# A fused attention and two-MLP kernel: q and k transposed by VectorE instead of TensorE, and w_out's two halves kept in DRAM

## Chip, cores and metric

The kernel runs on one core of a Trainium2 chip. The metric is device time in microseconds (us), the median of several executions; lower is better.

## The reference

```python
# attention: B=4, H=8, S=768, D=64; n_global=8, n_local=96
scores = scale * q @ k.T                       # per batch and head
rel = pos[:, None] - pos[None, :]
keep = (pos[None, :] < n_global) | ((rel >= 0) & (rel < n_local))
scores = where(keep, scores - slope[h] * dist, -1e9)
a = softmax(scores)                            # over keys
x = (a @ v)  -> reshaped to [B*S = 3072 tokens, H*D = 512]
# first MLP, 512 -> 2048 -> 512
h = x @ moe_w_in;  y = (h * cos(h)) @ moe_w_out
# second MLP, 512 -> 2048 -> 512
h = maximum(y @ moe2_w_in, 0);  out = (h * h) @ moe2_w_out
```

All arrays are float32. A query sees at most 96 keys behind it and the first 8 keys of the sequence.

## The kernel before

**Attention** is done in 48 groups. `place(G)` gives each group's batch `b`, its run `r` of 256 positions (three in a sequence) and its pair `j` of heads; four groups (the four pairs of heads) share a run. For a group, `load_qk` brings 256 rows of q and k for two heads with four DMAs into `raw`, positions on the partitions. TensorE turns them with four transposes of 128x128 into PSUM (`transpose_qk`, L593), and ScalarE copies the result into `kq` (`copy_qk`, L759), which holds for each pair of heads the first 8 keys, the 96 keys that precede the run, the run's 256 keys and its 256 queries, head dimension on the partitions. Before a run is overwritten, GpSimd moves the last 96 keys to the front (`move_tail`, L480); `copy_qk` waits for that (`tails_moved`). When `r` is 0 there is nothing to move, and ScalarE copies the first 8 keys to their places (L761).

Then, group by group: `scores` (TensorE, L615), `reduces` (VectorE, L962: adds the bias, takes the row's extreme), `exps` (ScalarE, L771), `invert` (VectorE, L968 and L970: one over the row sums), `normalise` (GpSimd, L487), `turn_probs` (TensorE, L633 and L636), `copy_probs` (ScalarE and VectorE, L741 to L743), `attend` (TensorE, L651), `round_x` (ScalarE, L786) and `low_x` (VectorE, L981). The last two split the result into a high and a low part for the MLP.

**The MLPs** work on six tiles of 512 tokens each. Both matrices and both activations are split in two (high, low), and each product is made from three matmuls. A step F is one block of 128 hidden units of one tile: `up(F)` has 12 matmuls (L557 to L559) and `down(F)` 12 (L576 to L578 in the first MLP, L581 to L583 in the second). There are 96 steps in each MLP, 16 in a tile. Between up and down, ScalarE copies the hidden block (`front`), VectorE computes angles (`angle`, L997 to L1003, first MLP only), ScalarE takes the sine, VectorE gates (`gate`), ScalarE rounds (`round_g`, L812) and VectorE forms the low part (`low_g`, L1017). GpSimd splits each step's 128 rows of w_out (`split_out`, L472 and L474) into one of three slots, anew for each tile, after a DMA of 256 KB (`load_w_out`); it waits until the down step that read the slot is done. In the first steps it also splits w_in (`split_in`, L463 and L465), and later the second MLP's w_in (`split_w2`), which goes through DRAM.

**Order.** Every engine's queue is written out by hand and runs in order; engines meet at semaphores. A prologue does the first 11 groups (`AHEAD`), a loop over G on each engine. GpSimd's loop is: `move_tail(G + 1)`, `normalise(G - 1)`, `split_in(G)` for G below 5 (`EARLY`). VectorE's is: `reduces(G)`, `biases(G + 1)` for the first few, `invert(G - 1)`, `copy_probs(G - 2)`, `low_x(G - 3)`. ScalarE's is: `copy_qk(G + 1)`, `exps(G)`, `copy_probs(G - 2)`, `round_x(G - 3)`. Then come pairs p of steps, F = 2p, in which the work of the groups G = p + 11 is woven, until p = 48. All DMAs are issued by SP, in order; a DMA whose wait isn't met holds up those behind it.

The program takes this path when n_local and n_global fit (here they do); a general path stands beside it.

Of the kernel before, what the change touches and what calls it, by code (L numbers as in the profile page):

```python
# [22 lines left out]
def build(nc, q, k, v, n_global, n_local, w1_in, w1_out, w2_in, w2_out, out):  # L23
# [39 lines left out]
    w2_dram = nc.dram_tensor("w2_dram", (FC, P, 2, KC, P), F32, kind="Internal").ap()  # L63
    y_dram = nc.dram_tensor("y_dram", (KC, P, TOK), F32, kind="Internal").ap()

    with ExitStack() as ctx:
# [17 lines left out]
        raw = sb("raw", [P, 3, 2, 2, 2 * D])  # L84
# [15 lines left out]
        with ExitStack() as lay:  # L100
            x_parts = [sb(f"x_parts{i}", [P, 2, KC, NT], F32R, lay) for i in range(2)]
            w_stage = sb("w_stage", [P, 2, KC, P], F32, lay)
            w_out_raw = sb("w_out_raw", [P, 2, DM], F32, lay)
            w_out_hi = sb("w_out_hi", [P, 3, DM], F32R, lay)
            w_out_lo = sb("w_out_lo", [P, 3, DM], F32R, lay)
# [36 lines left out]
        def turn_bank(G):  # L142
            return 6 if G <= AHEAD else 5

# [32 lines left out]
        qk_transposed = sem("qk_transposed")  # L177
        tails_moved = sem("tails_moved")
        qkT_copied = sem("qkT_copied")
# [21 lines left out]
        w_out_hi_ready = sem("w_out_hi_ready")  # L201
        w_out_ready = sem("w_out_ready")
# [29 lines left out]

        def tails(G):
            return sum(place(n)[1] > 0 for n in range(G + 1))

# [27 lines left out]
        def _(sp):  # L263
# [55 lines left out]
            def load_w_out(F):  # L319
                src, f = (w1_out if F < STEPS else w2_out), F % FC  # L320
                if F >= 2:
                    sp.wait_ge(w_out_ready, F - 1)
                sp.dma_start(w_out_raw[:, F % 2], src[P * f:P * f + P, :]).then_inc(w_out_loaded[F % 2], 16)

# [25 lines left out]
            def pair(p, window):  # L350
                F, G = 2 * p, p + AHEAD
                i, s = divmod(p, FC // 2)
                if window and G + 3 < GROUPS:
                    load_qk(G + 3)
                if window and G + 1 < GROUPS:
                    load_values(G + 1)
                for n in (F + 1, F + 2):
                    if STEPS - FC <= n < STEPS:
                        place_w2(n - (STEPS - FC))
                if W2_FROM <= p < W2_FROM + 2 * FC:  # L360
                    n, late = divmod(p - W2_FROM, 2)
# [12 lines left out]
                if F + 5 < STEPS_ALL:  # L374
                    load_w_out(F + 5)

# [26 lines left out]
            def general():  # L403
                sp.wait_ge(qk_loaded[0], 64)
# [33 lines left out]
        def _(pool):  # L438
# [28 lines left out]
            def split_out(F):  # L467
                pool.wait_ge(w_out_loaded[F % 2], 16 * (F // 2 + 1))
                if F >= 3:
                    pool.wait_ge(down_done, KC * (F - 2))  # L470
                row, hi, lo = w_out_raw[:, F % 2], w_out_hi[:, F % 3], w_out_lo[:, F % 3]
                pool.tensor_scalar(hi, row, 1.0, 1.0, ALU.mult, ALU.mult).then_inc(w_out_hi_ready, 1)  # L472
                pool.wait_ge(w_out_hi_ready, F + 1)
                pool.tensor_tensor(lo, row, hi.bitcast(F32), ALU.subtract).then_inc(w_out_ready, 1)  # L474
# [28 lines left out]
            def window():  # L503
                for G in range(AHEAD):
# [3 lines left out]
                    if G < EARLY:  # L508
                        split_in(G)
                normalise(AHEAD - 1)  # L510
# [9 lines left out]
            def general():  # L520
                pool.wait_ge(mask_steps, MASK_STEPS)
                pool.wait_ge(qk_loaded[0], 64)
# [16 lines left out]
        def _(pe):  # L539
# [22 lines left out]
            def down(F, window):  # L562
                i, f = divmod(F, FC)
                pe.wait_ge(w_out_ready, F + 1)
# [5 lines left out]
                for c in range(KC):  # L570
# [3 lines left out]
                    if i < TILES:  # L574
                        hi, lo = w_out_hi[:, F % 3, cols], w_out_lo[:, F % 3, cols]
# [3 lines left out]
                    else:  # L579
                        hi, lo = g_hi[:, F % 3, cols], g_lo[:, F % 3, cols]  # L580
                        pe.matmul(to, hi, w_out_hi[:, F % 3], start=one, stop=False)  # L581
                        pe.matmul(to, hi, w_out_lo[:, F % 3], start=False, stop=False)  # L582
                        last = pe.matmul(to, lo, w_out_hi[:, F % 3], start=False, stop=end)  # L583
                    last.then_inc(down_done, 1)

            def transpose_qk(G):
                pe.wait_ge(qk_loaded[G % 3], 64 * (G // 3 + 1))
                if 0 < G <= AHEAD:
                    pe.wait_ge(qkT_copied, G)
                if G > AHEAD:  # L590
                    pe.wait_ge(x_lo_ready, G - 2)
                for n in range(4):
                    last = pe.transpose(psum[:, turn_bank(G), P * n:P * n + P], raw[:, G % 3, n // 2, n % 2], ident[:])  # L593
                last.then_inc(qk_transposed, 1)

            def scores(G):
                b, r, j = place(G)
                pe.wait_ge(qkT_copied, G + 1)
# [40 lines left out]
            def attend(G):  # L639
# [4 lines left out]
                if 0 < G < AHEAD - 1:  # L644
                    pe.wait_ge(x_lo_ready, G)
# [11 lines left out]
            def pair(p, window):  # L657
# [8 lines left out]
                if window and G + 1 < GROUPS:  # L666
                    transpose_qk(G + 1)
# [8 lines left out]
            def window():  # L676
                transpose_qk(0)
                for G in range(AHEAD - 1):
                    scores(G)
                    transpose_qk(G + 1)  # L680
# [6 lines left out]
                transpose_qk(AHEAD)  # L687
# [61 lines left out]
        def _(act):  # L749

            def copy_qk(G):
                b, r, j = place(G)
                act.wait_ge(qk_transposed, G + 1)
                if r > 0:
                    act.wait_ge(tails_moved, tails(G))
                elif G >= PAIRS:
                    act.wait_ge(scores_ready, 2 * (G - PAIRS + 1))
                ends = kq[:, j, BACK:Q_AT + 2 * P].rearrange("p (a n) -> p a n", a=2)[:, :, GLOB:]
                last = act.copy(ends, psum[:, turn_bank(G)].rearrange("p (a n) -> p a n", a=2))  # L759
                if r == 0:  # L760
                    last = act.copy(kq[:, j].rearrange("p (a n) -> p a n", a=2)[:, :, 0:GLOB],  # L761
                                    psum[:, turn_bank(G), None, 0:GLOB].to_broadcast((P, 2, GLOB)))
                last.then_inc(qkT_copied, 1)
# [57 lines left out]
            def pair(p, window):  # L821
# [10 lines left out]
                if window and G + 1 < GROUPS:  # L832
                    copy_qk(G + 1)
# [19 lines left out]
            def window():  # L853
                act.wait_ge(consts_set, 2)
                copy_qk(0)
                for G in range(AHEAD - 1):
                    copy_qk(G + 1)
# [6 lines left out]
                copy_qk(AHEAD)  # L864
# [38 lines left out]
        def _(dve):  # L903
# [18 lines left out]

            masked = [0]
# [5 lines left out]

            dve.wait_ge(iotas_set, 8)  # L930
# [122 lines left out]
            def window():  # L1053
                biases(0)
                for G in range(AHEAD - 1):
                    reduces(G)
# [8 lines left out]
                low_x(AHEAD - 4)  # L1065
                reduces(AHEAD - 1)
# [107 lines left out]
```

## Time and profile before

| | |
|---|---|
| median of 3 runs | 1246.7 us (1246.59 to 1250.46) |
| profiled execution: its time | 1248.4 us |
| profiled execution: its span | 1246.6 us |
| TensorE busy | 1218.5 us, 98% of the span |
| VectorE, GpSimd, ScalarE busy | 736.8, 625.1, 559.6 us |
| mean granted TensorE clock | 0.999 |
| moved by DMA | 118.80 MB |

The span runs from the first to the last instruction of one profiled execution; its time is a little longer. Busy is the time in which an engine executes. Matmuls are pipelined: their durations overlap, so the distance between the starts of two of them says what one costs.

### The profile page before, as it was taken

The numbers are of one execution on the slowest core, as the hardware profiler recorded it, in microseconds if no ns is written. First come the engines' busy times: TensorE is split into PE (matmuls) and PEld (weight loads), VectorE is DVE, ScalarE is ACT, GpSimd is POOL, SyncE is SP. The second block draws the span as 40 slices with busy tenths as digits, with TensorE's granted clock in tenths as the row PEclk, the third lists the DMA queues.
The fourth block names the chain that finished last, engine by engine and source line by source line (L and its number), as shares of the span: only waits on it lengthen the run. The fifth ranks groups of instructions, "written<-read, shape, count | busy, mean of one in ns | idle before, by whom it ended". The sixth has DMA issues, their size and how long they took to land.

```text
span 1246.6 us, 18120 instructions
## 1 busy us (share of the span) xinstructions
PE 1218.5 (98%) x6240; PEld 991.6 (80%) x6240; DVE 736.8 (59%) x1434; ACT 559.6 (45%) x1164; POOL 625.1 (50%) x687
## 2 busy tenths in 40 slices
PE   5789999999999999999999999999999999999998
PEld 3667888887888877888888888888888888888887
DVE  6579988888878888788888933223323223223222
ACT  4656767666666666676433322222222222222211
POOL 4468966555666665666543433333334334333332
PEclk9999999999999999999999999999999999999999
DMA  4523434333433333342155441131131221311211
GB/s 122 146 70 102 110 101 137 97 89 92 146 97 104 124 89 104 112 133 84 54 148 177 138 138 52 51 111 51 51 116 46 81 89 49 113 51 51 78 50 60
DMA packets 150949, 118.80 MB, mean 95 GB/s; under 512 B 63680, under 2 KB 115008, under 8 KB 150848
## 3 DMA queue, kind: packets, MB, share of 16 engines
q1 hardware_dynamic: 150848, 117.55, 32.6%
q8 instruction: 52, 0.85, 0.3%
q14 instruction: 49, 0.40, 0.1%
HBM read 96.54 MB, written 20.97 MB: 94 GB/s over the span
## 4 chain that ended last, share of the span: by engine, by line
PE 94%; DVE 2%; ACT 1%; POOL 1%; DMA 1%; issue 1%; SPq 0%; DVEq 0%; ACTq 0%; POOLq 0%
PE psum L557 14%; PE psum L559 14%; PE psum L558 14%; PE psum L576 8%; PE psum L582 7%; PE psum L583 7%; PE psum L581 7%; PE psum L578 7%; PE psum L577 7%; PE psum L651 3%; PE psum L615 3%; PE psum L636 2%; PE psum L593 1%; ACT probs L771 1%; POOL probs L487 0%
## 5 line engine op out<-in xcount | busy, mean ns | idle before, releaser
L472 POOL TENSOR_SCALAR w_out_hi<-w_out_raw 128x512 fp32r<-128x512 f32 x192 | 136.5, 711 | 549.8 <-PE psum L583 312.6
L557 PE MATMUL psum<-x_parts,w_in_hi 128*128 128x512 f32 x768 | 302.9, 394 | 2.6 <-ACT hs L800 2.6
L559 PE MATMUL psum<-x_parts,w_in_lo 128*128 128x512 f32 x768 | 299.4, 390 | 0.0
L558 PE MATMUL psum<-x_parts,w_in_hi 128*128 128x512 f32 x768 | 298.8, 389 | 0.0
L474 POOL TENSOR_TENSOR w_out_lo<-w_out_raw,w_out_hi 128x512 fp32r<-128x512 f32 x192 | 264.2, 1376 | 16.0
L1017 DVE TENSOR_TENSOR g_lo<-act_a,g_hi 128x512 fp32r<-128x512 f32 x192 | 139.9, 729 | 187.1 <-ACT g_hi L812 181.7
L802 ACT ACTIVATE hs<-psum 128x512 f32<-128x512 f32 x96 | 57.4, 598 | 359.9 <-PE psum L559 359.9
L557 PEld LDWEIGHTS psum<-x_parts,w_in_hi 128*128 128x128 f32 x768 | 144.2, 188 | 32.0 <-issue 3.6
L559 PEld LDWEIGHTS psum<-x_parts,w_in_lo 128*128 128x128 f32 x768 | 144.2, 188 | 30.6
L558 PEld LDWEIGHTS psum<-x_parts,w_in_hi 128*128 128x128 f32 x768 | 144.4, 188 | 28.9
L576 PE MATMUL psum<-g_hi,w_out_hi 128*128 128x512 f32 x384 | 157.7, 411 | 0.5 <-issue 0.5
L578 PE MATMUL psum<-g_hi,w_out_lo 128*128 128x512 f32 x384 | 150.5, 392 | 0.0
L577 PE MATMUL psum<-g_lo,w_out_hi 128*128 128x512 f32 x384 | 149.8, 390 | 0.0
L581 PE MATMUL psum<-w_out_hi,g_hi 128*128 128x512 f32 x384 | 149.4, 389 | 0.0
L582 PE MATMUL psum<-w_out_lo,g_hi 128*128 128x512 f32 x384 | 149.4, 389 | 0.0
L583 PE MATMUL psum<-w_out_hi,g_lo 128*128 128x512 f32 x384 | 149.4, 389 | 0.0
L487 POOL TENSOR_SCALAR probs<-probs,row_inv 128x232 f32<-128x232 f32 (+1 forms) x192 | 128.0, 684 | 30.4 <-DVE row_inv L970 30.4
L812 ACT CAST g_hi<-act_a 128x512 fp32r<-128x512 f32 x192 | 118.6, 618 | 50.2 <-DVE act_a L1013 27.2
L800 ACT COPY hs<-psum 128x512 f32<-128x512 f32 x96 | 56.1, 584 | 158.5 <-PE psum L559 158.5
L1013 DVE TENSOR_TENSOR act_a<-hs 128x512 f32<-128x512 f32 x96 | 64.2, 687 | 89.3 <-ACT hs L802 89.3
L1009 DVE TENSOR_TENSOR act_a<-hs,act_a 128x512 f32<-128x512 f32 x96 | 76.2, 830 | 63.8 <-ACT act_a L806 63.7
L1001 DVE SCALAR_TENSOR_TENSOR act_a<-turns,hs 128x512 f32<-128x512 f32 x96 | 100.2, 1044 | 3.3
(76 smaller groups left out, 1657.6 us busy)
## 6 DMA issues: line engine op xcount, KB each, us to landing
w_out_raw<-in_moe_w_out_dram SPq DMA_DIRECT2D x192, 256.0 KB, 2.7
vals<-in_v_dram SPq DMA_DIRECT2D x80, 112.0 KB
w_stage<-in_moe_w_in_dram SPq DMA_DIRECT2D x32, 256.0 KB, 3.0
w_dram<-w_stage SPq DMA_DIRECT2D x16, 512.0 KB, 3.3
raw<-in_k_dram SPq DMA_DIRECT2D x96, 64.0 KB, 2.5
raw<-in_q_dram SPq DMA_DIRECT2D x96, 64.0 KB, 2.3
y_dram<-y_stage SPq DMA_DIRECT2D x24, 256.0 KB, 3.7
x_raw<-y_dram SPq DMA_DIRECT2D x6, 1024.0 KB, 5.1
```

Source lines behind the costliest of these rows:

```text
L472: pool.tensor_scalar(hi, row, 1.0, 1.0, ALU.mult, ALU.mult).then_inc(w_out_hi_ready, 1)
L474: pool.tensor_tensor(lo, row, hi.bitcast(F32), ALU.subtract).then_inc(w_out_ready, 1)
L557: pe.matmul(to, hi, x[:, 0, c], start=(c == 0), stop=False)
L558: pe.matmul(to, hi, x[:, 1, c], start=False, stop=False)
L559: last = pe.matmul(to, lo, x[:, 0, c], start=False, stop=(c == KC - 1))
L576: pe.matmul(to, hi, g_hi[:, F % 3], start=one, stop=False)
L577: pe.matmul(to, hi, g_lo[:, F % 3], start=False, stop=False)
L578: last = pe.matmul(to, lo, g_hi[:, F % 3], start=False, stop=end)
L581: pe.matmul(to, hi, w_out_hi[:, F % 3], start=one, stop=False)
L582: pe.matmul(to, hi, w_out_lo[:, F % 3], start=False, stop=False)
L583: last = pe.matmul(to, lo, w_out_hi[:, F % 3], start=False, stop=end)
L1017: dve.tensor_tensor(g_lo[:, F % 3], act_a[:, F % 4], g_hi[:, F % 3].bitcast(F32), ALU.subtract).then_inc(g_lo_ready, 1)
```

## The change

- `load_qk` fills `raw` in another layout: eight DMAs a group instead of four, each for one head's half of the head dimension on 32 partitions, with 256 positions as eight blocks of 32 columns.
- `transpose_qk` on TensorE and `copy_qk` on ScalarE are gone. `turn_qk` on VectorE transposes k and q with one instruction each, in blocks of 32x32, from `raw` straight into `kq`; for `r` = 0 a third instruction copies the first 8 keys. In the prologue and in the pairs it does group G + 1 ahead of `reduces(G)`; `turn_qk(0)` stands ahead of the masks.
- In the pairs, GpSimd moves the keys back for group G + 2 instead of G + 1, ahead of the splits. In the prologue's loop it is still G + 1.
- w_out is split only in each MLP's first tile (`is_split`). There SP stores both halves of a step into `w_out_dram`; for the other five tiles it fetches them, 512 KB a step, into the same three slots, after `down_done` of the step that used the slot.

```diff
-        raw = sb("raw", [P, 3, 2, 2, 2 * D])
+        raw = sb("raw", [P, 3, 2, PAD])
...
     def load_qk(G):
         b, r, j = place(G)
         if G >= 3:
-            sp.wait_ge(qk_transposed, G - 2)
+            sp.wait_ge(qk_turned, G - 2)
         for i, src in enumerate((k, q)):
             for h in range(2):
-                rows = src[b, 2 * j + h, PAD * r:PAD * r + PAD]
-                sp.dma_start(raw[:, G % 3, i, :, D * h:D * h + D], rows.rearrange("(t p) d -> p t d", p=P))\
-                  .then_inc(qk_loaded[G % 3], 16)
+                rows = src[b, 2 * j + h, PAD * r:PAD * r + PAD].rearrange("(n p) (a d) -> a p n d", p=32, a=2)
+                for a in range(2):
+                    at = 64 * h + 32 * a
+                    sp.dma_start(raw[at:at + 32, G % 3, i].rearrange("p (n d) -> p n d", d=32), rows[a]).then_inc(qk_loaded[G % 3], 16)
...
+    def is_split(F):
+        return F % STEPS < FC
...
+    def store_w_out(F):
+        if is_split(F):
+            sp.wait_ge(w_out_ready, splits(F) + 1)
+            sp.dma_start(w_out_dram[F // STEPS, F % FC], w_out[:, F % 3].bitcast(F32)).then_inc(w_out_stored[F % 3], 16)
+
+    def fetch_w_out(F):
+        if F >= STEPS_ALL or is_split(F):
+            return
+        sp.wait_ge(down_done, KC * (F - 2))
+        for s in range(3) if F % STEPS == FC else (F % 3,):
+            sp.wait_ge(w_out_stored[s], 16 * slot_splits(F - F % 3 + s if F % 3 >= s else F - F % 3 + s - 3))
+        sp.dma_start(w_out[:, F % 3].bitcast(F32), w_out_dram[F // STEPS, F % FC]).then_inc(w_out_fetched[F % 3], 16)
...
     # SP, pair(p)
+                store_w_out(F)
+                store_w_out(F + 1)
+                fetch_w_out(F + 2)
                 if F + 4 < STEPS_ALL:
                     load_w_out(F + 4)
...
+                fetch_w_out(F + 3)
...
     # GpSimd, pair(p)
+                if window and G + 2 < GROUPS:
+                    move_tail(G + 2)
                 if F + 2 < STEPS_ALL:
                     split_out(F + 2)
-                if window and G + 1 < GROUPS:
-                    move_tail(G + 1)
...
     # TensorE: transpose_qk and its calls removed
-            for n in range(4):
-                last = pe.transpose(psum[:, turn_bank(G), P * n:P * n + P], raw[:, G % 3, n // 2, n % 2], ident[:])
...
     # ScalarE: copy_qk and its calls removed
...
     # VectorE
+    def turn_qk(G):
+        b, r, j = place(G)
+        dve.wait_ge(qk_loaded[G % 3], 128 * (G // 3 + 1))
+        if r > 0:
+            dve.wait_ge(tails_moved, tails(G))
+        elif G >= PAIRS:
+            dve.wait_ge(scores_ready, 2 * (G - PAIRS + 1))
+        dve.transpose(kq[:, j, K_AT:G_B], raw[:, G % 3, 0]).then_inc(k_turned, 1)
+        dve.transpose(kq[:, j, Q_AT:Q_AT + PAD], raw[:, G % 3, 1]).then_inc(qk_turned, 1)
+        if r == 0:
+            dve.wait_ge(k_turned, G + 1)
+            dve.tensor_copy(kq[:, j].rearrange("p (a n) -> p a n", a=2)[:, :, 0:GLOB],
+                            kq[:, j, None, K_AT:K_AT + GLOB].to_broadcast((P, 2, GLOB))).then_inc(globals_moved, 1)
...
     # VectorE: in pair(p), ahead of angle(F + 2); in the prologue, ahead of reduces(G)
+                if window and G + 1 < GROUPS:
+                    turn_qk(G + 1)
```

## Rows read from the trace of the kernel before

**Rows 1.** The page: busy time (share of the span) and instructions of each engine.

```profile
PE 1218.5 (98%) x6240; PEld 991.6 (80%) x6240; DVE 736.8 (59%) x1434; ACT 559.6 (45%) x1164; POOL 625.1 (50%) x687
```

**Rows 2.** Busy time by window: length, each engine's busy us, PEclk, DMA share, GB/s.

```profile
50.00:60.00 10.00, 6.96 (x60) 5.64 (x59) 3.94 (x18) 4.14 (x14) 2.83 (x8) 0.83 0.56 141
...
119.00:133.00 14.00, 14.00 (x80) 11.16 (x79) 13.36 (x27) 9.37 (x22) 13.22 (x13) 1.00 0.35 96
...
640.00:700.00 60.00, 60.00 (x266) 49.71 (x265) 54.55 (x71) 22.02 (x39) 24.30 (x22) 1.00 0.64 188
700.00:900.00 200.00, 200.00 (x884) 165.65 (x883) 70.55 (x101) 50.87 (x90) 75.02 (x74) 1.00 0.26 79
```

**Rows 3.** Timeline of TensorE: start us, us, then the instruction.

```profile
395.97 0.50 PE L576 MATMUL psum<-g_hi,w_out_hi 128*128 128x512 f32 x1
...
398.60 0.39 PE L578 MATMUL psum<-g_hi,w_out_lo 128*128 128x512 f32 x1
...
399.49 0.39 PE L558 MATMUL psum<-x_parts,w_in_hi 128*128 128x512 f32 x1
...
405.43 0.39 PE L578 MATMUL psum<-g_hi,w_out_lo 128*128 128x512 f32 x1
...
405.88 0.39 PE L558 MATMUL psum<-x_parts,w_in_hi 128*128 128x512 f32 x1
...
410.48 0.50 PE L576 MATMUL psum<-g_hi,w_out_hi 128*128 128x512 f32 x1
...
846.00 0.39 PE L581 MATMUL psum<-w_out_hi,g_hi 128*128 128x512 f32 x1
...
856.88 0.39 PE L581 MATMUL psum<-w_out_hi,g_hi 128*128 128x512 f32 x1
```

**Rows 4.** Timeline of VectorE in the same pair.

```profile
403.69 0.71 DVE L1017 TENSOR_TENSOR g_lo<-act_a,g_hi 128x512 fp32r<-128x512 f32 x1
```

**Rows 5.** Groups by form: count, busy us, mean ns, idle us before and who ended it.

```profile
L472 POOL TENSOR_SCALAR w_out_hi<-w_out_raw 128x512 fp32r<-128x512 f32 x192 | 136.5, 711 | 549.8 <-PE psum L583 312.6 <-PE psum L578 237.2
...
L593 PE MATMUL psum<-ident,raw 128*128 128x128 f32 x192 | 31.6, 290 | 8.8 <-issue 7.2 <-DMA raw<-in_q_dram 1.4
...
L743 DVE COPY probsT<-psum 116x512 f32<-116x512 f32 x32 | 21.8, 680 | 3.0 <-PE psum L651 2.8 <-PE psum L636 0.2
...
L742 DVE COPY probsT<-psum 116x256 f32<-116x256 f32 x16 | 6.6, 410 | 0.0
```

**Rows 6.** Timeline of the prologue, GpSimd and VectorE.

```profile
33.76 0.62 POOL L463 TENSOR_SCALAR w_in_hi<-w_stage 128x512 fp32r<-128x512 f32 x1
...
34.50 0.39 DVE L962 CUSTOM_DVE_ANT_0 probs<-psum,bias 128x232 f32<-128x232 f32 x1
...
35.67 0.26 POOL L480 COPY kq<-kq 128x96 f32<-128x96 f32 x1
...
35.77 0.19 DVE L968 TENSOR_SCALAR row_sum<-row_sum 128x4 f32<-128x4 f32 x1
...
36.38 1.76 POOL L487 TENSOR_SCALAR probs<-probs,row_inv 128x232 f32<-128x232 f32 x4 [0.44 <-DVE row_inv L970]
```

**Rows 7.** Timeline: invert of groups 1 and 8 on VectorE, first matmul of the MLP.

```profile
21.31 0.18 DVE L970 RECIPROCAL row_inv<-row_sum 128x4 f32<-128x4 f32 x1
...
52.41 0.18 DVE L970 RECIPROCAL row_inv<-row_sum 128x4 f32<-128x4 f32 x1
...
60.62 0.48 PE L557 MATMUL psum<-x_parts,w_in_hi 128*128 128x512 f32 x1
```

**Rows 8.** SP's DMA issues by line: ns min/median/max, first and last start; landing from issue.

```profile
L274 SPq DMA_DIRECT2D raw<-in_q_dram x96: 462/469/480, 2.6 to 547.0; - x96
...
DMA to landing us min/median/max: 1.9/2.3/3.4
...
L287 SPq DMA_DIRECT2D vals<-in_v_dram x16: 367/368/469, 11.0 to 467.7; - x16
```

**Rows 9.** Timeline of ScalarE in the prologue: the copy of group 4's q and k.

```profile
26.98 0.58 ACT L759 COPY kq<-psum 128x512 f32<-128x512 f32 x1 [4.20 <-POOL kq L480]
```

More of the change, by code:

```diff
@@ L63, in build @@
     w2_dram = nc.dram_tensor("w2_dram", (FC, P, 2, KC, P), F32, kind="Internal").ap()
+    w_out_dram = nc.dram_tensor("w_out_dram", (2, FC, P, 2, DM), F32, kind="Internal").ap()
     y_dram = nc.dram_tensor("y_dram", (KC, P, TOK), F32, kind="Internal").ap()
@@ L103, in build @@
             w_out_raw = sb("w_out_raw", [P, 2, DM], F32, lay)
-            w_out_hi = sb("w_out_hi", [P, 3, DM], F32R, lay)
-            w_out_lo = sb("w_out_lo", [P, 3, DM], F32R, lay)
+            w_out = sb("w_out", [P, 3, 2, DM], F32R, lay)
             hs = sb("hs", [P, 4, NT], F32, lay)
@@ L201, in build @@
         w_out_hi_ready = sem("w_out_hi_ready")
+        w_out_stored = [sem(f"w_out_stored{i}") for i in range(3)]
+        w_out_fetched = [sem(f"w_out_fetched{i}") for i in range(3)]
         w_out_ready = sem("w_out_ready")
@@ L231, in v_count, with starts, splits, slot_splits @@
             return 16 * sum(v_dmas(n) for n in range(G % 3, G + 1, 3))
+        def starts(G):
+            return sum(place(n)[1] == 0 for n in range(G + 1))
         def tails(G):
             return sum(place(n)[1] > 0 for n in range(G + 1))
+        def is_split(F):
+            return F % STEPS < FC
+        def splits(F):
+            return sum(is_split(n) for n in range(F))
+        def slot_splits(F):
+            return sum(is_split(n) for n in range(F % 3, F, 3))
+        def slot_fetches(F):
+            return sum(not is_split(n) for n in range(F % 3, F, 3))
         def x_lo_wait(eng, i, window):
@@ L319, in load_w_out @@
             def load_w_out(F):
[L320 to L323 removed]
+                if not is_split(F):
+                    return
+                src, f, n = (w1_out if F < STEPS else w2_out), F % FC, splits(F)
+                if n >= 2:
+                    sp.wait_ge(w_out_ready, n - 1)
+                sp.dma_start(w_out_raw[:, F % 2], src[P * f:P * f + P, :]).then_inc(w_out_loaded[F % 2], 16)
+            def store_w_out(F):
[4 more added lines that the diff above has]
+                if F >= STEPS_ALL or is_split(F):
+                    return
+                sp.wait_ge(down_done, KC * (F - 2))
+                for s in range(3) if F % STEPS == FC else (F % 3,):
+                    sp.wait_ge(w_out_stored[s], 16 * slot_splits(F - F % 3 + s if F % 3 >= s else F - F % 3 + s - 3))
+                sp.dma_start(w_out[:, F % 3].bitcast(F32), w_out_dram[F // STEPS, F % FC]).then_inc(w_out_fetched[F % 3], 16)
             def load_x(n):
@@ L467, in split_out @@
             def split_out(F):
-                pool.wait_ge(w_out_loaded[F % 2], 16 * (F // 2 + 1))
+                if not is_split(F):
+                    return
+                n = splits(F)
+                pool.wait_ge(w_out_loaded[F % 2], 16 * (n // 2 + 1))
                 if F >= 3:
                     pool.wait_ge(down_done, KC * (F - 2))
-                row, hi, lo = w_out_raw[:, F % 2], w_out_hi[:, F % 3], w_out_lo[:, F % 3]
+                    pool.wait_ge(w_out_stored[F % 3], 16 * slot_splits(F))
+                row, hi, lo = w_out_raw[:, F % 2], w_out[:, F % 3, 0], w_out[:, F % 3, 1]
                 pool.tensor_scalar(hi, row, 1.0, 1.0, ALU.mult, ALU.mult).then_inc(w_out_hi_ready, 1)
-                pool.wait_ge(w_out_hi_ready, F + 1)
+                pool.wait_ge(w_out_hi_ready, n + 1)
                 pool.tensor_tensor(lo, row, hi.bitcast(F32), ALU.subtract).then_inc(w_out_ready, 1)
@@ L509, in window @@
                         split_in(G)
+                move_tail(AHEAD + 1)
                 normalise(AHEAD - 1)
@@ L563, in down @@
                 i, f = divmod(F, FC)
-                pe.wait_ge(w_out_ready, F + 1)
+                if is_split(F):
+                    pe.wait_ge(w_out_ready, splits(F) + 1)
+                else:
+                    pe.wait_ge(w_out_fetched[F % 3], 16 * (slot_fetches(F) + 1))
                 pe.wait_ge(g_lo_ready, F + 1)
@@ L574, in down @@
                     if i < TILES:
-                        hi, lo = w_out_hi[:, F % 3, cols], w_out_lo[:, F % 3, cols]
+                        hi, lo = w_out[:, F % 3, 0, cols], w_out[:, F % 3, 1, cols]
                         pe.matmul(to, hi, g_hi[:, F % 3], start=one, stop=False)
@@ L580, in down @@
                         hi, lo = g_hi[:, F % 3, cols], g_lo[:, F % 3, cols]
-                        pe.matmul(to, hi, w_out_hi[:, F % 3], start=one, stop=False)
-                        pe.matmul(to, hi, w_out_lo[:, F % 3], start=False, stop=False)
-                        last = pe.matmul(to, lo, w_out_hi[:, F % 3], start=False, stop=end)
+                        pe.matmul(to, hi, w_out[:, F % 3, 0], start=one, stop=False)
+                        pe.matmul(to, hi, w_out[:, F % 3, 1], start=False, stop=False)
+                        last = pe.matmul(to, lo, w_out[:, F % 3, 0], start=False, stop=end)
                     last.then_inc(down_done, 1)
[L586 to L591, printed above, removed]
-                for n in range(4):
-                    last = pe.transpose(psum[:, turn_bank(G), P * n:P * n + P], raw[:, G % 3, n // 2, n % 2], ident[:])
-                last.then_inc(qk_transposed, 1)
             def scores(G):
                 b, r, j = place(G)
-                pe.wait_ge(qkT_copied, G + 1)
+                pe.wait_ge(qk_turned, G + 1)
+                if r == 0:
+                    pe.wait_ge(globals_moved, starts(G))
                 if 2 <= G < AHEAD:
@@ L749, in _ @@
         def _(act):
[L751 to L763, printed above, removed]
             def exps(G):
@@ L928, in then @@
                 dve.wait_ge(mask_steps, masked[0])
+            turn_qk(0)
             dve.wait_ge(iotas_set, 8)
@@ L1055, in window @@
                 for G in range(AHEAD - 1):
+                    turn_qk(G + 1)
                     reduces(G)
@@ L1065, in window @@
                 low_x(AHEAD - 4)
+                turn_qk(AHEAD)
                 reduces(AHEAD - 1)
```

24 lines of the change are left out of this document (7 added, 17 removed).

## The prediction

> **What bounds the kernel now.** The page comes first: it says which engine is full. TensorE is busy for 98% of the span, the next engine, VectorE, for 59% [rows 1]. A busy share can hide waits, so the windows come next [rows 2]: in the second MLP (700 to 900) TensorE is busy 200.00 of 200 us, while VectorE stands at 71 and GpSimd at 75. Before 60 us it is not full: 6.96 of 10 us, with some 4 us or less on each other engine. There the wait between engines sets the pace, and the granted clock falls to 0.83, so part of that stretch ran at the lower of the two levels, 1.2 GHz, after TensorE had stood idle. So the kernel has three parts: a prologue bound by a loop of waits (to 60.6 us, where the first hidden matmul starts [rows 7]), 37 pairs of steps with attention bound by TensorE, and the rest, bound by TensorE's matmuls alone.
>
> The timeline of TensorE [rows 3] gives the price of its own work. Two successive first down matmuls stand at 395.97 and 410.48: a pair with attention takes 14.51 us and has no gap that counts. The same step of two pairs of the second MLP stands at 846.00 and 856.88: 10.88 us a pair.
>
> **What leaves TensorE.** Four transposes of q and k in each pair. From the last down matmul at 398.60 to the second up matmul at 399.49, over the transposes, it is 0.89 us; the same change from down to up without them, 405.43 to 405.88, takes 0.45 [rows 3]. So a group's transposes cost 0.44 us, though their row says 290 ns each [rows 5]: they overlap. Of the 48 groups, 12 are turned in the prologue, where TensorE waits anyway, and 36 in pairs; the first of these pairs is bound by VectorE and ScalarE, not TensorE. 35 x 0.44 = 15.4 us off. This is the whole gain I see. ScalarE loses 48 copies of 0.58 us [rows 9], hidden: it is busy 45% of the span [rows 1].
>
> **What goes to VectorE.** Two transposes of 128x256 a group. No row shows one. The nearest is the copy of 116x256 at 410 ns; the copy of 116x512, 680 ns, is twice the elements and the upper bound; half of the 410 would be the lower one [rows 5]. VectorE's successive operations overlap by some 0.05, so I take 0.37 each, 0.75 us a group. As a rule the Trainium skill has a front-end that turns 32x32 blocks at one element a cycle and lane ("Vector Engine (DVE) Microarchitecture Reference", section 3.8); it would leave this term as it is, and no run here shows it yet. Another page gives 311 ns for 128x128 of two-byte data ("VectorE: DVE Perf Modes", section The three transpose paths); doubled, that would be an estimate of 0.6 for one of these and would put the sum some 5 us higher.
>
> In the pairs this has cover. In an attention pair g_lo for the next first down step is started at 403.69 and ends at 404.40; that step starts at 410.48 [rows 3, 4]: 6.1 us of slack. After the first tile GpSimd's splits of w_out are gone as well. In the first tile they stay, and VectorE is busy 13.36 of 14 us [rows 2]. With 0.75 more it needs 14.1 a pair where TensorE will need 13.5 to 14.1: at most 0.6 us short, over six pairs less than the slack. I take nothing, and up to 4 us for the range.
>
> **The prologue, where I think most of the gain is lost.** There VectorE gets turn_qk(G+1) ahead of reduces(G). It waits for the keys moved back (tails_moved), and behind it in VectorE's queue stand reduces(G) and invert(G-1). GpSimd does move_tail(G+1) only after normalise(G-2) and split_in(G-1), and normalise(G-2) waits for invert(G-2). The edit "a pair early" is in the pairs; in the prologue's loop move_tail keeps its place. Before, the copy on ScalarE took this wait (4.20 us for group 4 [rows 9]), and reduces went on beside it. Now a loop closes once a group:
> invert to normalise, 35.77 to 36.38: 0.61; normalise 1.76; the move 0.26; two transposes 0.75; reduces, 34.50 to 35.77: 1.27 [rows 6]. Sum 4.65 us. While split_in is in the loop, 33.76 to 35.67 or 1.91 us more: 6.56 [rows 6].
> Tails start with group 4, so three turns of the loop are at 6.56 and four at 4.65: 38.3 us from invert(1) to invert(8). Before it was 52.41 - 21.31 = 31.1 [rows 7]. That is 7.2 us lost. Ahead of invert(1), turn_qk(0) waits for eight loads in place of none (about 1.4 us), and four turns of 0.75 stand before it: 4.4. From invert(8) to the first hidden matmul it took 60.62 - 52.41 = 8.2; with VectorE this late, TensorE's steps for groups 6 and 7 are ready earlier, and I count 6.5: 1.7 back. Prologue +9.9, and 0.5 for turn_qk(11) ahead of reduces(10) and turn_qk(12) ahead of the first angles, most of which the copy taken off ScalarE pays: +10.4.
>
> **The queue of SP.** A group's q and k are eight loads in place of four. A load whose two sides are both in pieces takes 469 ns to issue, one with pieces on the DRAM side alone 368 [rows 8]; the new ones are of the second kind. With 0.04 between them, eight take 3.3 us, at the worst 4.1, and the values of a group 1.5. 4.8 a group is about the loop's 4.65 and below it while split_in and its load count; the load of group 10 is issued at some 55 and landed 2.3 later [rows 8], before the loop wants it at 62. At 0.51 each it is issued at 62 and landed at 65: 2 to 3 us more. I take none. The Trainium skill speaks against such cuts: transfers to disjoint parts of the partitions share the same 16 engines, one 128-partition transfer is advised ("DMA: Bandwidth & Descriptors", section Rules for kernel authors). The rows here can't tell yet; by that rule the price is the queue time just given.
>
> **w_out.** 160 of 192 splits go from GpSimd, the first half of each at 711 ns. Its row shows 549.8 us of idle time before them, all of it waiting for TensorE [rows 5]: GpSimd was ahead, so this is worth nothing on the path. In their place come 32 stores and 160 fetches of 512 KB for loads of 256 KB. A fetch is issued once the down step that used its slot is done, two and a half steps or 13 us ahead of its use, and lands within about 4. The densest stretch, 640 to 700, moved 188 GB/s at a DMA share of 0.64 with TensorE busy 60.00 of 60 [rows 2]; 256 KB more each 5.4 us adds 48 GB/s, which still fits. If a fetch did come late, each step of 5.4 us would show it. Behind SP's waits for down_done stand only the next pair's loads, for groups two and three ahead.
>
> **Sum.** -15.4 + 10.4 = -5.0 us. The profiled execution took 1248.4 us (span 1246.6), the median of the runs is 1246.7; the same 5 us off the median gives 1242.
>
> **Rivals.**
> Cheap prologue (0.22): the loop doesn't close as tightly, or a transpose takes near 0.3, and the prologue costs 3 to 6 us. For it: VectorE is busy only 3.94 of 10 us at the prologue's end [rows 2]. Against it: the order in its queue. Time 1234 to 1238.
> The gain is eaten wholly (0.20): SP's issues at 0.51 and a TensorE at 1.2 GHz through more of the prologue, which stands idle more (the clock fell in 50 to 60 already [rows 2]), bring the prologue to 13 to 17 us: 1244 to 1249, about no change.
> Slow transposes (0.14), the case on the other side: one takes 0.68 [rows 5]. The prologue has ten loops of 0.6 more, +6; in the first tile VectorE needs 13.36 + 1.4 of 14 us, 1 us or more a pair beyond TensorE over six pairs, of which the slack takes most, +2 to 4. Time 1250 to 1253. It decides from about 0.65 us a transpose.
> Nothing gained in the pairs (0.04): some other engine sets 14.5 too. The slack [rows 4] and the shorter pairs without attention speak against it. 1252 to 1257.
>
> **How the numbers follow.** My case, 1239 to 1245, has 0.40. About 0.3% (3.7 us) is what a measurement can tell. Faster than 1243.0: the cheap prologue, 0.28 of my 0.40 and a little of the third: 0.52. Within it: 0.34. Slower than 1250.4: 0.14. The range runs from 1235 to 1251 and leaves out the far ends.
>
> **What would show it.** Right: attention pairs of 14.07 us in place of 14.51; no row of the transposes on TensorE; VectorE's transposes at 0.35 to 0.42; VectorE waiting in the prologue on the move of keys, 2 us and more for groups 4 to 6; the first hidden matmul at about 70.5; the pairs of the second MLP unchanged at 10.88. Wrong: a first hidden matmul before 66 or after 75, a pair that stays above 14.2, VectorE's transposes above 0.6, or TensorE waiting for fetched w_out.

## The result and the profile after

The changed kernel takes 1252.66 us, the median of 11 runs (1250.78 to 1253.63); the kernel before, run on the same chips, takes 1248.60 (11 runs, 1246.59 to 1251.21). The ratio is 1.0031, 95% interval 1.0023 to 1.0039: slower by 0.3%, about 4 us, where 5 us faster were forecast. The profiled execution has a span of 1249.8 us where before it was 1246.6, so 3.2 us more are to be found in the traces.

The page answers to [rows 1], and four windows to [rows 2].

```profile
PE 1204.5 (96%) x6048; PEld 978.2 (78%) x6048; DVE 704.8 (56%) x1546; ACT 535.9 (43%) x1100; POOL 253.4 (20%) x367
```

```profile
50.00:60.00 10.00, 7.88 (x70) 6.37 (x70) 6.00 (x25) 4.87 (x19) 3.95 (x10) 0.84 0.48 98
119.00:133.00 14.00, 13.85 (x79) 10.84 (x78) 13.67 (x29) 8.87 (x19) 9.81 (x11) 1.00 0.58 163
640.00:700.00 60.00, 60.00 (x266) 49.69 (x265) 41.79 (x73) 23.07 (x39) 0.00 (x0) 1.00 0.75 234
700.00:900.00 200.00, 200.00 (x884) 165.66 (x883) 65.61 (x102) 51.49 (x91) 32.02 (x32) 1.00 0.43 149
```

TensorE is busy for 14 us less and yet the span is longer: it stands idle for 45.3 us (1249.8 - 1204.5), where before it was 28.1. From 640 on it is full as before, with the DMA share at 0.75 and 234 GB/s: the fetches of w_out cost it nothing.

The timeline of TensorE answers to [rows 3, 7]: the first hidden matmul, first down matmuls of pairs 1, 7, 38 and two in the middle, and two of the second MLP.

```profile
73.19 0.47 PE L598 MATMUL psum<-x_parts,w_in_hi 128*128 128x512 f32 x1
...
107.02 0.50 PE L620 MATMUL psum<-g_hi,w_out 128*128 128x512 f32 x1
...
197.62 0.50 PE L620 MATMUL psum<-g_hi,w_out 128*128 128x512 f32 x1
...
398.14 0.47 PE L620 MATMUL psum<-g_hi,w_out 128*128 128x512 f32 x1
...
412.19 0.47 PE L620 MATMUL psum<-g_hi,w_out 128*128 128x512 f32 x1
...
626.08 0.50 PE L620 MATMUL psum<-g_hi,w_out 128*128 128x512 f32 x1
...
843.81 0.39 PE L625 MATMUL psum<-w_out,g_hi 128*128 128x512 f32 x1
...
854.69 0.39 PE L625 MATMUL psum<-w_out,g_hi 128*128 128x512 f32 x1
```

An attention pair takes 412.19 - 398.14 = 14.05 us, a pair of the second MLP 10.88 as before. With the same points read from the two traces, the span comes apart into stages (us; the first row ends at the first hidden matmul, the others at the first down matmul of the step named):

| stage | before | after | difference | forecast |
|---|---|---|---|---|
| prologue, to the first hidden matmul | 60.62 | 73.19 | +12.57 | +10.4 |
| steps 0 to 2 | 35.13 | 33.83 | -1.30 | 0 |
| steps 2 to 14 (rest of the first tile) | 84.97 | 90.60 | +5.63 | -2.6 |
| steps 14 to 76 | 442.11 | 428.46 | -13.65 | -12.8 |
| from step 76 on | 623.74 | 623.74 | 0.0 | 0 |
| sum | 1246.57 | 1249.82 | +3.25 | -5.0 |

The forecast column shares the predicted 15.4 us over the pairs that had transposes, six in the third row and 29 in the fourth. The surprise is in the third: the first tile was to win 2.6 us and lost 5.6.

**The first tile.** GpSimd's timeline from 156 to 173 us shows what is new there.

```profile
158.32 1.61 POOL L514 TENSOR_TENSOR w_out<-w_out_raw,w_out 128x512 fp32r<-128x512 f32 x1
164.27 0.72 POOL L512 TENSOR_SCALAR w_out<-w_out_raw 128x512 fp32r<-128x512 f32 x1 [4.34 <-DMA w_out_dram<-w_out]
...
171.05 1.15 POOL L499 TENSOR_SCALAR w_in_hi<-w_stage 128x512 fp32r<-128x512 f32 x1
172.29 1.59 POOL L501 TENSOR_TENSOR w_in_lo<-w_stage,w_in_hi 128x512 fp32r<-128x512 f32 x1
```

The bracket is the idle time before an instruction and what ended it: `split_out` (L512) waits 4.34 us until an earlier store of its slot has landed. SP's timeline shows why the store is late.

```profile
154.67 2.87 SPq L292 DMA_DIRECT2D raw<-in_k_dram  x4
157.58 1.93 SPq L292 DMA_DIRECT2D raw<-in_q_dram  x4
159.56 0.45 SPq L306 DMA_DIRECT2D vals<-in_v_dram  x1
160.05 0.36 SPq L307 DMA_DIRECT2D vals<-in_v_dram  x1
160.45 0.31 SPq L308 DMA_DIRECT2D vals<-in_v_dram  x1
160.81 0.36 SPq L309 DMA_DIRECT2D vals<-in_v_dram  x1
161.21 0.82 SPq L347 DMA_DIRECT2D w_out_dram<-w_out  x2
```

The pair's twelve loads of q, k and v are issued ahead of its two stores, 6.5 us of queue, and only then do the stores go out. Behind `split_out` in GpSimd's queue stand `normalise` and the next pair's `split_in`, and TensorE's chain of waits from 95 to 200 us ends there.

```profile
POOL w_out L512 <- DMA w_out_dram<-w_out: 21.1, 5, 6.3
...
PE psum L598 <- POOL w_in_lo L501: 5.7, 3, 3.0
```

(Engine, line, what it waited for: us in total, times, longest.) GpSimd waits 21.1 us for stores, TensorE 5.7 us for the low half of w_in that GpSimd then makes late. Neither pair of waits exists in the trace of before.

A part of this loss is TensorE's clock. After its wait of 2.95 us for `w_in_lo`, which ends at 171.13, the granted clock is 0.50, the lower of the two levels:

```profile
171.50:174.80 3.30, 3.30 (x9) 2.63 (x8) 2.92 (x3) 0.73 (x2) 3.22 (x4) 0.50 0.67 213
```

In that stretch up matmuls start 0.43 us apart where elsewhere they stand 0.23 apart; eight of them make an estimate of 1.6 us, inside the 5.6 of this stage. Before, and with the transposes alone, the clock doesn't fall in this stage.

**The prologue.** VectorE's timeline at the transposes of groups 4, 5 and 10:

```profile
30.95 0.45 DVE L942 STREAM_TRANSPOSE kq<-raw 128x256 f32<-128x256 f32 x1 [3.56 <-POOL kq L520]
31.32 0.40 DVE L943 STREAM_TRANSPOSE kq<-raw 128x256 f32<-128x256 f32 x1
...
37.11 0.45 DVE L942 STREAM_TRANSPOSE kq<-raw 128x256 f32<-128x256 f32 x1 [2.20 <-POOL kq L520]
...
58.83 0.45 DVE L942 STREAM_TRANSPOSE kq<-raw 128x256 f32<-128x256 f32 x1 [1.05 <-DMA raw<-in_q_dram]
```

Two transposes start 0.37 us apart. At first they wait for the keys moved back, as forecast, and later for the loads. SP's timeline of one group, without w_in, and its whole list of waits from 20 to 73 us:

```profile
53.70 1.79 SPq L292 DMA_DIRECT2D raw<-in_k_dram  x4
55.53 1.93 SPq L292 DMA_DIRECT2D raw<-in_q_dram  x4
57.50 0.45 SPq L306 DMA_DIRECT2D vals<-in_v_dram  x1
57.99 0.36 SPq L307 DMA_DIRECT2D vals<-in_v_dram  x1
58.40 0.31 SPq L308 DMA_DIRECT2D vals<-in_v_dram  x1
58.75 0.36 SPq L309 DMA_DIRECT2D vals<-in_v_dram  x1
59.16 1.79 SPq L292 DMA_DIRECT2D raw<-in_k_dram  x4
```

```profile
SPq L292 <- DVE kq L943: 0.6, 1, 0.6
```

A group's issues take 59.16 - 53.70 = 5.46 us, and in 53 us SP stood still for 0.6; before, it waited for 6.9 of the 41 us from 20 to 61. It has become an engine that is full: nothing it does can start earlier.

### The profile page after: what moved, and what is told of

Read it like the earlier page. It is cut to its first block, busy times and chain, and to the rows that moved or that the text cites. A ratio compares the mean times of both kernels' runs of the same rounds, so it can differ in the third digit from the quotient of the medians.

```text
span 1249.8 us, 17695 instructions
## 1 busy us (share of the span) xinstructions
PE 1204.5 (96%) x6048; PEld 978.2 (78%) x6048; DVE 704.8 (56%) x1546; ACT 535.9 (43%) x1100; POOL 253.4 (20%) x367
## 4 chain that ended last, share of the span: by engine, by line
PE 88%; SPq 5%; POOL 2%; DMA 1%; issue 1%; ACT 1%; DVE 1%; POOLq 0%; DVEq 0%; ACTq 0%
PE psum L598 13%; PE psum L600 13%; PE psum L599 13%; PE psum L627 7%; PE psum L625 7%; PE psum L626 7%; PE psum L620 7%; PE psum L622 6%; PE psum L621 6%; SPq L292 4%; PE psum L687 3%; PE psum L651 3%; PE psum L672 2%; POOL probs L527 1%; DMA w_out_dram<-w_out 1%
## 5 line engine op out<-in xcount | busy, mean ns | idle before, releaser
L1044 DVE TENSOR_TENSOR g_lo<-act_a,g_hi 128x512 fp32r<-128x512 f32 x192 | 153.2, 798 | 197.7 <-ACT g_hi L829 194.7
L527 POOL TENSOR_SCALAR probs<-probs,row_inv 128x232 f32<-128x232 f32 (+1 forms) x192 | 90.9, 492 | 339.8 <-DVE row_inv L997 339.8
L620 PE MATMUL psum<-g_hi,w_out 128*128 128x512 f32 x384 | 157.7, 411 | 0.5 <-issue 0.5
L622 PE MATMUL psum<-g_hi,w_out 128*128 128x512 f32 x384 | 150.4, 392 | 0.0
L621 PE MATMUL psum<-g_lo,w_out 128*128 128x512 f32 x384 | 149.8, 390 | 0.0
L625 PE MATMUL psum<-w_out,g_hi 128*128 128x512 f32 x384 | 149.4, 389 | 0.0
L626 PE MATMUL psum<-w_out,g_hi 128*128 128x512 f32 x384 | 149.4, 389 | 0.0
L627 PE MATMUL psum<-w_out,g_lo 128*128 128x512 f32 x384 | 149.4, 389 | 0.0
L788 ACT ACTIVATE probs<-probs,row_min 128x232 f32<-128x232 f32 (+1 forms) x192 | 88.8, 464 | 31.3 <-DVE row_min L989 30.9
L620 PEld LDWEIGHTS psum<-g_hi,w_out 128*128 128x128 f32 x384 | 72.1, 188 | 19.9 <-issue 7.3
L622 PEld LDWEIGHTS psum<-g_hi,w_out 128*128 128x128 f32 x384 | 72.0, 188 | 16.1
```

The source lines that it names most:

```text
L527: pool.tensor_scalar(probs[:, G % 3, u, 0:w], probs[:, G % 3, u, 0:w], row_inv[:, G % 3, u:u + 1], 1.0, ALU.mult, ALU.mult).then_inc(probs ...
L620: pe.matmul(to, hi, g_hi[:, F % 3], start=one, stop=False)
L621: pe.matmul(to, hi, g_lo[:, F % 3], start=False, stop=False)
L622: last = pe.matmul(to, lo, g_hi[:, F % 3], start=False, stop=end)
L625: pe.matmul(to, hi, w_out[:, F % 3, 0], start=one, stop=False)
L626: pe.matmul(to, hi, w_out[:, F % 3, 1], start=False, stop=False)
```

## The experiments

Each ratio is to the kernel before as it ran beside that experiment (medians of 1247.30, 1248.79 and 1248.39 us), with its 95% interval; where a stage is named, its points are those of the table, read from one profiled execution.

### The transposes alone

```diff
     def is_split(F):
-        return F % STEPS < FC
+        return True
...
-                store_w_out(F)
-                store_w_out(F + 1)
...
-                    pool.wait_ge(w_out_stored[F % 3], 16 * slot_splits(F))
```

> The q and k part alone: w_out is split in every tile as before the change, no stores, no fetches. Theory (split_out in the first tile waits for its slot's store to land): pairs 2 to 5 fall from 13.8 to 18.4 us to about 14.0, GpSimd no longer waits for a store, the prologue stays at 73.2 us, and the time is 8 us under the changed kernel, about 1244.5. Rival (VectorE is the bound of the first tile, with the transposes at 0.8 us more a pair): pairs 2 to 5 stay at 15 us and more, here even with GpSimd's splits beside VectorE in every tile; time 1251 to 1256. Rival (little by both): 1248.

Measured: 1249.18 us, ratio 1.0006 (0.9997 to 1.0015). The first hidden matmul stands at 74.79. From step 2 to 14 it takes 195.61 - 110.12 = 85.49 us: 5.1 less than in the changed kernel, and 0.5 more than before where 2.6 less was due. So the q and k part alone comes out even, and of the 8.2 us by which the first tile missed its forecast, 5.1 belong to w_out and 3.1 to the transposes. The theory was right on GpSimd's waits and too high on the time: it had 8 us under the changed kernel, and the ratios are 0.25% or 3.1 us apart. The pairs came to 14.0 to 14.6 us instead of 14.0, steps 0 to 2, at 35.33 us, lack what the changed kernel gains there (33.83), and the prologue is 1.6 us later.

### w_out in DRAM alone

```diff
 # TensorE's transposes, ScalarE's copies and four loads a group as before; from the change:
+            w_out = sb("w_out", [P, 3, 2, DM], F32R, lay)
...
+                store_w_out(F)
+                store_w_out(F + 1)
+                fetch_w_out(F + 2)
```

> The w_out part alone on the kernel before: transposes stay on TensorE, q and k come in four loads. Theory (a loop over SP's queue, the store's landing and GpSimd's splits sets 15.6 us a pair in the changed kernel's first tile): SP has 2 us less in each turn of the loop, so it closes at about 13.6, under the 14.5 of a pair, and the first tile costs 0 to 2 us; prologue unchanged at 60.6; time within 0.2% of before. Rival (a store's landing costs its 4 us wherever it stands): the first tile is 5 to 8 us longer. Rival (w_out's fetches are a cost or a gain in later tiles): pairs differ from 14.51 and 10.88.

Measured: 1253.08 us, ratio 1.0038 (1.0026 to 1.0051): slower by 0.4% by itself, more than the theory's 0.2%. The prologue is 61.30, near that of before. From step 2 to 14 it takes 88.53 us, 3.6 more than before, between the theory's 0 to 2 and the rival's 5 to 8. The pairs of steps 8 and 10 take 15.95 and 15.85 us where before they took 14.06 and 14.07, and GpSimd waits for stores:

```profile
POOL w_out L509 <- DMA w_out_dram<-w_out: 20.2, 5, 8.2
```

### The stores ahead of the loads

```diff
+                store_w_out(F)
+                store_w_out(F + 1)
                 if window and G + 3 < GROUPS:
                     load_qk(G + 3)
...
-                store_w_out(F)
-                store_w_out(F + 1)
```

> The changed kernel with the two stores of w_out at the head of SP's pair, ahead of eight loads of q and k and four of v. Theory (the store is issued late in SP's queue, 5.7 us after it could be): GpSimd finds the store landed, pairs 2 to 5 come to about 14.0 and the time falls by 5 to 8 us, to 1245 to 1248. Rival (VectorE is the bound there): pairs stay above 15, no change beyond 1 us.

Measured: 1248.62 us, ratio 1.0011 (1.0002 to 1.0019). Steps 2 to 14 take 85.49 us, as with the transposes alone. The waits of GpSimd and TensorE from 95 to 200 us:

```profile
POOL probs L527 <- DVE row_inv L997: 22.2, 8, 6.1
...
PE psum L598 <- ACT hs L817: 3.2, 5, 1.1
PE psum L672 <- DVE row_min L989: 2.7, 1, 2.7
```

No wait is put down to a store any more (one idle time of 3.95 us before the last split is put down to nothing), and the clock no longer falls in this stage. The 5.1 us that w_out cost from step 2 to 14 were the place of the stores in SP's queue, the slower clock behind the waits included. The whole run gains less than those 5.1, and less than the 5 to 8 of the theory: the span falls by 3.3 us (1249.82 to 1246.55), the ratio by 0.20% or 2.5 us. Steps 0 to 2 are 1.4 us longer than with the late stores (35.27 against 33.83) and the prologue 0.4.

The same reordering was made in the kernel that has the w_out part alone:

> The kernel before with w_out kept in DRAM (as in the run of that part alone), but each pair's two stores issued ahead of the pair's loads of q, k and v. Theory (the late stores are the whole loss of this part, 3.8 us): pairs 8 and 10, which took 15.95 and 15.85 us, come back to about 14.1, and the time is that of the kernel before within 1.5 us, since the splits taken off GpSimd are worth nothing on the path. Rival (the 512 KB stores and fetches cost something by themselves, or the lighter GpSimd is worth something): the time stays 2 us or more above, or falls 2 us or more below.

Measured: 1248.99 us, ratio 1.0004 (0.9992 to 1.0016). Steps 8 and 10 are back at 14.06 and 14.07 us. The theory held: w_out in DRAM, with its stores in time, is worth nothing and costs nothing that can be measured. The 1.5 us more of span in the profiled execution (1248.0 against 1246.6) lie in steps 0 to 2, where the granted clock is 0.50 from 91.4 to 94.7 us; in the kernel before it is 1.00 there.

### The keys moved a group earlier in the prologue

```diff
             for G in range(AHEAD):
-                move_tail(G + 1)
+                move_tail(G + 2)
...
-                move_tail(AHEAD + 1)
```

> The changed kernel with move_tail(G + 2) in place of G + 1 in the prologue's loop too. Theory (the GpSimd loop sets the prologue for groups 4 to 7, SP's issues from group 8 on): VectorE's waits of 3.56, 2.20, 2.14 and 0.38 us on the move go, but a part comes back as waits for the loads, which SP issues at 5.4 to 5.9 us a group; the first hidden matmul moves from 73.2 to 70 to 72, the time falls by 1 to 3 us. Rival (the loop alone is the cost, as predicted): it moves to about 65, the time falls by 7 or 8. Rival (SP alone sets it): no change.

Measured: 1252.63 us, ratio 1.0040 (1.0027 to 1.0053); the first hidden matmul at 73.27, where the changed kernel has it at 73.19. VectorE's waits from 20 to 73 us:

```profile
DVE kq L941 <- DMA raw<-in_q_dram: 11.3, 8, 3.4
DVE x_parts L1007 <- ACT x_parts L802: 8.3, 8, 2.6
```

In the changed kernel this was 8.3 us for the keys and 3.8 for the loads, 12.1 together; with the keys in time it is 11.3 for the loads alone. The loop through GpSimd can be taken out and the prologue doesn't move, as the rival had it. What is left to set it is SP's queue or the loads' own time in the DMA engines; the next two experiments part these.

### Eight loads in the kernel before

```diff
-                        sp.dma_start(raw[:, G % 3, i, :, D * h:D * h + D], rows.rearrange("(t p) d -> p t d", p=P))
+                        for t in range(2):
+                            at = PAD * r + P * t
+                            sp.dma_start(raw[:, G % 3, i, t, D * h:D * h + D], src[b, 2 * j + h, at:at + P])
```

> The kernel before with one thing added: q and k of a group come in eight loads of 32 KB in place of four of 64 KB, in the old layout; transposes stay on TensorE, w_out as before. Theory (SP's issuing sets the prologue once there are eight): if one is issued in 0.37 to 0.4 us, a group takes SP 4.7 us and more, and the first hidden matmul moves from 60.6 to 62 to 66; if it is 0.51, to 68 to 72. The time is later by the same and nothing else changes: pairs stay at 14.51, the first tile has slack. Rival (the place of turn_qk on VectorE is the cost, not the loads): at most 0.5 us later.

Measured: 1261.61 us, ratio 1.0102 (1.0086 to 1.0118). Nothing is changed but that each load is cut in two, and the first hidden matmul goes from 60.62 to 73.93: 13.3 us, and 13.3 us in the span. That is past the 68 to 72 of the theory's dearer case. The view of one line shows these loads, and who waits for them up to 74 us:

```profile
L275 SPq DMA_DIRECT2D raw<-in_q_dram x52: 432/432/1452, 3.6 to 73.8; - x52
...
  PEld psum L594: 29.3, 11
  PE psum L594: 24.2, 10
```

One takes 432 ns to issue with 32 KB in it; with 64 KB it was 469 [rows 8]. The half costs nearly what the whole did. From 20 to 74 us SP waits for 1.0 us only. Added up from its timeline to the first hidden matmul, SP's issues take 45.4 us in the kernel before, 64.7 in the changed one and 65.2 here.

### The q loads issued by ScalarE

```diff
+                for G in (1, 2):
+                    load_rows(act, G, 1)
                 act.wait_ge(consts_set, 2)
                 for G in range(AHEAD - 1):
+                    if G:
+                        load_rows(act, G + 2, 1)
                     exps(G)
```

`load_rows(eng, G, i)` issues the four loads of q (i = 1) or k from the engine named; SP issues those of k, and for group 0 and from group 12 on both. This kernel has the stores first and the keys moved a group early as well.

> Stores first, the keys moved a pair early in the prologue too, and the four q loads of groups 1 to 11 issued from ScalarE's queue in place of SP's. Theory (after the loads of q and k became eight, SP's issuing time, 5.4 us a group, sets the prologue): SP needs 3.4 us a group, the prologue's first hidden matmul moves from 73.6 to 63 to 67, and the time falls 7 to 10 us under the kernel with stores first, to 1239 to 1242, which beats the kernel before. Rival (the loads are slow in the DMA engines, not in the queue): VectorE waits for loads as before and the prologue stays above 71. Rival (the order of VectorE's queue is the next bound): 67 to 70, time 1243 to 1246.

Measured: 1237.54 us, ratio 0.9913 (0.9899 to 0.9927). The first hidden matmul stands at 62.22. It beats the kernel before and the changed one, by more than the theory had. SP's issues up to there are back at 45.7 us, with 20.0 on ScalarE's queue, and VectorE's waits for loads from 20 to 62 us are 1.8 us: the same loads are no longer late, so it was the issuing and not the DMA engines. Against the kernel with only the keys early, 11 us of prologue are gone. Whether the q loads on ScalarE do this without the keys moved early was not tried.

With turn_qk(G + 1) behind reduces, biases and invert in VectorE's queue in addition:

> As the one with q on ScalarE's queue, and in the prologue turn_qk(G + 1) stands behind reduces(G), biases and invert(G - 1) on VectorE. Theory (with SP's queue relieved, VectorE's wait for loads still holds up reduces behind it): another 1 to 3 us off, first hidden matmul at 61 to 64, time 1237 to 1240. Rival (SP's queue was all): no further change. Rival (scores(G + 1) are then late, since they wait for turn_qk): 1 to 2 us slower than with turn_qk first.

Measured: 1237.30 us, ratio 0.9905 (0.9891 to 0.9919), the same within the intervals. In its profiled execution the first hidden matmul is later, 65.53, but that execution is the longest of the five (1240.28 us) and doesn't speak for the median. This order on VectorE brings nothing to be seen.

The last kernel leaves w_out as it was before:

> VectorE's transposes alone, w_out split for every tile as in the kernel before, with the prologue's move of the keys a group early and the q loads of groups 1 to 11 issued from ScalarE's queue. Theory (w_out in DRAM is worth nothing; the gain is the transposes off TensorE with the prologue's loss taken away): the first hidden matmul at about 62, and a time within 1.5 us of the 1237.5 of the version with w_out in DRAM. Rival (the lighter GpSimd of the w_out part carries some of that version's gain): 1240 or more, with TensorE or VectorE waiting for GpSimd in the pairs with attention.

Measured: 1238.24 us, ratio 0.9920 (0.9898 to 0.9941). The first hidden matmul stands at 62.46. The theory held: the whole gain is that of the transposes taken off TensorE; w_out in DRAM adds nothing that can be told.

## Why the prediction was wrong

Its sum missed the profiled execution by 8.2 us. Three terms that it put at nothing are at fault: w_out (5.1 us), VectorE in the first tile (3.1) and SP's queue, for which the prologue is 2.2 over its forecast; 2.2 us came back in steps 0 to 2 and in the later pairs. No single one decides: with w_out left out, the transposes alone still come out even, not 5 us faster.

- **w_out, the first step that failed.** "This is worth nothing on the path" held for the splits taken away. But the prediction costed the stores by their share of the DMA engines and looked for a wait only at the fetches, and never at the new wait in `split_out` for its slot's store, nor at what stands ahead of that store in SP's queue. That is the wait it was to name, with what is queued behind it: normalise, `split_in`, and TensorE's up step. From step 2 to 14 it cost 5.1 us, and moving the two stores gave the 5.1 back there; over the whole run they gave 2.5 (by the ratios) to 3.3 (by the spans).
- **VectorE in the first tile, the second.** "I take nothing, and up to 4 us for the range": it was 3.1. VectorE is busy 13.67 of 14 us (13.36 before [rows 2]), and the pairs of the kernel with the transposes alone take 14.0 to 14.6 us where TensorE needs 13.5 to 14.1. That this part belongs to the transposes is shown, since it stays with w_out untouched; that VectorE's full queue is how it comes about is read from the busy share, and from its waits, which in that kernel are 0.6 us in all from 95 to 200 us (before, 7.9); it wasn't tested apart.
- **The prologue and SP's queue, the third: the size about right, the engine wrong.** Forecast +10.4, measured +12.57. The steps came out in the places named: invert(1) 5.4 us later (4.4 forecast); from invert(1) to invert(8) 66.46 - 26.71 = 39.75 (38.3 forecast); from there 6.7 to the first hidden matmul (6.5 forecast). The turns with `split_in` took 6.2 to 6.4 us, near the 6.56, and the next 4.62, as summed; but the last three took 5.35 to 5.48 instead of 4.65, which is SP's 5.46 a group. Two limits lay side by side, and only the experiments could part them: without the GpSimd loop nothing changed, with the eight loads alone, VectorE's queue as before, all of the loss was there. So the waits of the loop were there as described, but they weren't what the prologue paid for, and that their sum came near the loss is luck. "I take none" for SP's queue was the error: an issue was put at 368 ns, from the loads of v, and is 451, with 0.49 from one to the next. The split by pieces that led to the 368 isn't borne out: the eight loads in the old layout have neither side in pieces and take 432. The Trainium skill has the rule for the cure, that issuing from several engines "only saves sequencer issue time" ("DMA: Bandwidth & Descriptors", section Rules for kernel authors). The trace agrees, and here that time was the bound: 11 us of prologue.
- **Steps 0 to 2** were 1.3 us shorter, which the prediction didn't have. It goes with the late stores: with the stores first, or without any, these steps take 35.3 us, and TensorE's one wait for `reduces` there is 2.7 us where in the changed kernel it is 1.3. With w_out in DRAM alone they are not shorter than before (35.70), but there the clock fell within them; against the same kernel with the stores first (36.71) they are 1.0 shorter. Why a late store brings `reduces` forward stays open.
- **TensorE's gain in the pairs was right:** 14.05 us a pair where 14.07 was forecast, and 13.65 us over the 29 pairs after the first tile, 0.47 each where 0.44 was forecast.
- **The transposes on VectorE were right:** rows of 0.40 and 0.45 us, 0.37 us from one start to the next. By the Trainium skill's one element a cycle and lane ("Vector Engine (DVE) Microarchitecture Reference", section 3.8) the term stayed as it was, and the trace bears that out; the estimate of 0.6 from the other page of the Trainium skill ("VectorE: DVE Perf Modes", section The three transpose paths) isn't borne out.
- **The fetches were right:** no engine waits for one, and the second MLP's pairs stay at 10.88.

Of the rivals, the one in which the gain is eaten wholly comes nearest: SP's issues at near 0.5 us, and a prologue of 13 us. The granted clock did fall further, to 0.59 in the stretch from 40 to 50 us where before it was 1.00, TensorE having stood idle more; but the kernel before with eight loads had 0.81 there and lost as much, and in both SP had next to no wait that a faster TensorE could have ended sooner. So the clock is hardly what the prologue paid for, though that is argued and wasn't tested. What that rival lacked is the first tile, which put the time past its 1249. The measured 1252.66 lies in the 1250 to 1253 of the slow transposes, by luck: at 0.40 and 0.45 us they weren't slow.

## What to carry to other kernels

Cost a DMA twice: by its bytes and by its time in the queue that issues it, here 0.3 to 0.5 us each and hardly less for half the bytes. When a change cuts loads into more pieces, add up the issues of one turn and set them against the turn's length before anything else. Where a buffer gets a second reader, such as a store, its next writer waits for it, so issue that store ahead of the loads that nobody waits for yet.

## What the runs showed of the hardware

- **An issue costs its queue nearly the same for half the bytes.** 432 to 451 ns for 32 KB, 469 for 64 KB [rows 8]. Two queues issue side by side: with q from ScalarE the same loads took 472 ns there, and both streams ran at once.
- **GpSimd's work slowed VectorE's.** With w_out in DRAM VectorE does 43 us of transposes more and is busy for 704.8 us, where it was 736.8 [rows 1]. By form, the same instruction of `angle` takes 730 ns in the changed kernel (first row) and 880 with the transposes alone, where GpSimd still splits (second row):

```profile
L1028 DVE SCALAR_TENSOR_TENSOR act_a<-turns,hs 128x512 f32<-128x512 f32 x96 | 70.1, 730 | 3.3
```

```profile
L1025 DVE SCALAR_TENSOR_TENSOR act_a<-turns,hs 128x512 f32<-128x512 f32 x96 | 84.5, 880 | 3.3
```

In the kernel with w_out in DRAM alone VectorE is busy for 666.4 us, 70 less than before, with its own work unchanged; not every row gains, and one of 128x512 (`act_a<-hs,act_a`) goes from 830 to 917 ns. The Trainium skill says that GpSimd's interfaces to SBUF are shared with VectorE ("GPSIMD Engine Reference", section 1. Specifications); the rows agree, as far as the splits are what took this time: the same runs move more by DMA as well. It brought no time here, since VectorE isn't the bound once the first tile is over.
- **The DMA engines took far more than they had before.** 177.5 MB in place of 118.8, at 234 GB/s and a share of 0.75 between 640 and 700 us, without one wait of TensorE.
